# Turning the keys with packed matmuls in place of transposes, in a kernel of attention and two feed-forward layers

## The reference

```python
for t in range(S):
    cur = np.einsum('bhd,bhe->bhde', u[None] * kt, vt)
    y[:, :, t] = np.einsum('bhd,bhde->bhe', rt, state + cur)
    state = wt[:, :, :, None] * state + np.einsum('bhd,bhe->bhde', kt, vt)
```

## Time and profile before

| | |
|---|---|
| median of 3 runs | 1017.5 us (1017.02 to 1018.01) |
| profiled execution | 1017.5 us |
| its span | 1015.7 us |
| TensorE, matmuls | 994.5 us busy, 98% of the span |
| TensorE, weight loads | 971.7 us, 96% |
| vector engine | 559.8 us, 55% |
| scalar engine | 288.6 us, 28% |
| GpSimd | 24.4 us, 2% |
| mean granted TensorE clock | 0.998 |

### The profile page before, as it was taken

How to read it: one execution, slowest core, us unless ns; L and a number is a source line. 1 busy time by engine, 2 the same in 40 slices (tenths; PEclk the granted TensorE clock), 3 DMA queues, 4 the chain that set the end, 5 groups by cost and what they waited for, 6 DMA issues and landing times.

```text
span 1015.7 us, 27744 instructions
## 1 busy us (share of the span) xinstructions
PE 994.5 (98%) x11776; PEld 971.7 (96%) x11776; DVE 559.8 (55%) x1170; ACT 288.6 (28%) x604; POOL 24.4 (2%) x24
## 2 busy tenths in 40 slices
PE   5899999999999999999999999999999999999998
PEld 5799999999999999999999999999999999999998
DVE  7686655655656646556432437555545454555554
ACT  3435314223242241331222334222121222222212
POOL 4500000000000000000000000000000000000000
PEclk9999999999999999999999999999999999999999
DMA  6644401312113013110020413010101010101000
GB/s 162 167 135 120 117 14 35 109 30 64 53 29 92 25 31 91 52 38 2 26 60 1 138 35 125 1 47 1 47 1 47 1 46 0 46 4 43 15 11 24
DMA packets 42130, 52.96 MB, mean 52 GB/s; under 512 B 5152, under 2 KB 42016, under 8 KB 42016
## 3 DMA queue, kind: packets, MB, share of 16 engines
q1 hardware_dynamic: 40624, 51.04, 17.3%
q10 hardware_dynamic: 1392, 0.25, 0.2%
HBM read 39.48 MB, written 9.44 MB: 48 GB/s over the span
## 4 chain that ended last, share of the span: by engine, by line
PE 96%; DVE 1%; issue 1%; ACT 0%; ACTq 0%; DMA 0%; SPq 0%; DVEq 0%
PE products L166 18%; PE products L167 16%; PE products L168 16%; PE acc L168 12%; PE acc L166 12%; PE acc L167 12%; PE products L694 5%; PE products L736 1%; PE products L752 1%; PE products L671 1%; PE products L708 1%; PE products L721 1%; DMA x_parts<-f_y 0%; DVE k_in L927 0%; DVE a_sb L944 0%
## 5 line engine op out<-in xcount | busy, mean ns | idle before, releaser
L166 PE MATMUL products<-x_parts,weights_hi 128*128 128x384 f32 x576 | 200.9, 349 | 4.1 <-DMA x_parts<-f_y 1.9
L167 PE MATMUL products<-x_parts,weights_hi 128*128 128x384 f32 x576 | 194.2, 337 | 0.0
L168 PE MATMUL products<-x_parts,weights_lo 128*128 128x384 f32 x576 | 193.9, 337 | 0.0
L1235 DVE TENSOR_SCALAR leaky_low<-products,leaky_al 128x384 f32<-128x384 f32 x128 | 79.0, 617 | 169.4 <-PE products L168 169.3
L1095 DVE TENSOR_TENSOR g_sb<-a_g,products 128x384 f32<-128x384 f32 x96 | 53.2, 554 | 191.4 <-issue 129.5
L1182 ACT ACTIVATE leaky_g_hi<-leaky_g_sb 128x384 fp32r<-128x384 f32 x128 | 67.2, 525 | 295.0 <-DVE leaky_g_sb L1240 295.0
L514 ACT ACTIVATE g_hi<-g_sb 128x384 fp32r<-128x384 f32 x96 | 50.3, 524 | 254.1 <-DVE g_sb L1095 254.1
L166 PEld LDWEIGHTS products<-x_parts,weights_hi 128*128 128x128 f32 x576 | 108.1, 188 | 8.9 <-issue 5.3
L167 PEld LDWEIGHTS products<-x_parts,weights_hi 128*128 128x128 f32 x576 | 108.2, 188 | 0.0
L168 PEld LDWEIGHTS products<-x_parts,weights_lo 128*128 128x128 f32 x576 | 108.2, 188 | 0.0
L168 PE MATMUL acc<-g_hi,weights_lo 128*128 128x384 f32 x288 | 97.5, 338 | 0.0
(11 more groups left out here) (85 smaller groups left out, 1747.7 us busy)
## 6 DMA issues: line engine op xcount, KB each, us to landing
k_in<-in_k_dram SPq DMA_DIRECT2D x16, 336.0 KB, 3.9
r_in<-in_r_dram SPq DMA_DIRECT2D x16, 336.0 KB, 4.8
stage<-in_w_out_dram SPq DMA_DIRECT2D x14, 384.0 KB, 3.1
w_v<-in_v_dram SPq DMA_DIRECT2D x16, 288.0 KB, 3.5
y_dram<-x_in SPq DMA_DIRECT2D x8, 576.0 KB, 3.0
x_in<-y_dram SPq DMA_DIRECT2D x8, 576.0 KB, 4.4
out_dram<-leaky_out_sb SPq DMA_DIRECT2D x7, 576.0 KB, 3.3
stage<-in_w_dram SPq DMA_DIRECT2D x10, 336.0 KB, 3.8
```

The lines of the kernel that those rows point to most:

```text
L166: pe.matmul(out, w_hi, x_hi, start=first, stop=False)
L167: pe.matmul(out, w_hi, x_lo, start=False, stop=False)
L168: return pe.matmul(out, w_lo, x_hi, start=False, stop=last)
L1235: dve.tensor_scalar(self.low[f % 2][:, :], h, 0.0, self.al[:, f:f + 1], ALU.min, ALU.mult).then_inc(self.low_ready, 1)
```

## The change

The keys of a duo and stream were turned by six transposes, each of 112 channels x 128 positions against an identity of 112x112, giving 128 x 112 columns of PSUM, with three chunks in each of two banks. They are now turned by 24 ordinary matmuls: for each chunk, head and half, the 48x64 block of keys is the stationary operand, and a 48x48 identity on the same rows the moving one; the result is 64 positions x 48 columns. Each head has its own bank, with its chunks next to each other. The scalar engine's two copies of a stream therefore go by head and read 288 contiguous columns, where they had gone by half of the chunks and skipped the rows between the heads. The identity is loaded with two DMAs, one for the rows of each head, in place of one.

```diff
-        ident, leaf_mask = sb("ident", [ROWS, ROWS]), sb("leaf_mask", [P, BLOCK])
+        ident, leaf_mask = sb("ident", [P, D]), sb("leaf_mask", [P, BLOCK])
...
-                    for unit in range(2):
-                        copy(view(k_scratch[j], D * HALF * unit, [[D, HALF], [D * CH, 2], [1, D]], P),
-                             view(products, stream_bank(j, unit), [[ROWS, HALF], [64, 2], [1, D]], P)).then_inc(copied, 1)
+                    for hd in range(2):
+                        copy(view(k_scratch[j], D * CH * hd, [[1, D * CH]], P),
+                             view(products, stream_bank(j, hd), [[1, D * CH]], P)).then_inc(copied, 1)
...
-                act.dma_start(ident[:, :], constants[0:ROWS, 0:ROWS]).then_inc(ident_loaded, 16)
+                for hd in range(2):
+                    rows = slice(64 * hd, 64 * hd + 64)
+                    act.dma_start(ident[rows, :], constants[rows, 64 * hd:64 * hd + D]).then_inc(ident_loaded, 16)
...
-                        at = stream_bank(j, c // HALF) + ROWS * (c % HALF)
-                        last = pe.transpose(products[:, at:at + ROWS], k_in[j][:, c * P:(c + 1) * P], ident[:, :])
+                        for hd in range(2):
+                            for par in range(2):
+                                last = pe.matmul(view(products, stream_bank(j, hd) + D * c, [[1, D]], BLOCK, BLOCK * par),
+                                                 key_blocks(k_in[j], hd, c, par), ident[64 * hd:64 * hd + D, :], start=True, stop=True)
...
-                        pe.wait_ge(ident_loaded, 16)
+                        pe.wait_ge(ident_loaded, 32)
```

## The result

The changed kernel takes 1022.99 us (median of 5 runs, 1022.52 to 1023.82) against 1018.01 us for the kernel before in the same series. The ratio is 1.0052 with a 95% interval of 1.0041 to 1.0064: slower by 5.3 us, 4.2 to 6.5. Forecast were 4.3 us and 1021.8 us. The sign and the mechanism behind the start hold. The median of the five is 0.2 us inside the upper end of the range, 1023.2 us; the median of all 14 executions of the changed kernel in this series, 1023.37 us, lies 0.2 us above it.

A forecast was written before the change was run, and what follows sets the result against it. TensorE was taken as the bound, with 96% of the last-ending chain. Seven packets at 4.1 us, 0 for duo 0, copies and loads, and 0.25 us irregular waits made 4.3 us on 1017.5, so 1021.8 us; range 1019.8 to 1023.2 us.

The forecast's parts named there:

- the packet is paced by its weight columns: Turning packets of duos 1 to 7: 64 weight columns make each 2.10 us instead of 1.515, together 4.1 us more.
- Rival B: Turning packets behind the start: smaller moving operands give 1.93 us each, 2.9 us more in all, 1020.4 us; chance 0.08.
- E: Turning packets: quadrants overlap fully, each costs 1.57 us like the last level, 0.4 us more, 1017.9 us; chance 0.04.
- Copies, the second DMA for the identity, SBUF: Key copies hidden behind large matmuls, second identity load covered by 17 us, smaller tile without effect: 0 us.
- Irregular slots: Overlong packets between 50 and 512 us: a tenth more small instructions adds 0.25 us, bounds 0 and 1.9 us.
- Rival C: Gated stage: more waits on issue, two of the worst long packets met, 6.0 us more, 1023.5 us; chance 0.06.
- Duo 0: 0 us, with +0.4 as the upper bound: Turning packet in the start: costs the same as its transposes, 2.78 against 2.84 us; bounds -0.1 and +0.4 us.
- Rival D: Start's clock shifts: slow stretch at 34 to 38 us moves, half returns, 1.7 us, giving 1020.1 us; chance 0.06.
- The slow stretch of the earlier trace: TensorE from 34 to 38 us at mean granted clock 0.57; its disappearance would show the forecast wrong.
- The second half of D: Start: matmuls raise the clock where transposes do not, a further 1.2 us comes off, 1018.9 us; chance 0.02.

The follow-up runs named there:

- the two kernels with fewer columns: Changed kernel streaming only 16 of 48 moving columns, and changed kernel loading only 32 of 64 weight columns; single times 1026.82 and 1020.61 us.
- the partial kernels: Kernel before with packed matmuls only in duos 1 to 7 (ratio 1.0038), only in duo 0 (1.0025), or everywhere but stream 0 of duo 0 (1.0045).
- duo 0 alone: Kernel before with only duo 0's keys turned by packed matmuls; 1020.47 us, ratio 1.0025, and in a second series 1020.53 us, ratio 1.0021.
- transposes by head: Changed kernel with its packed matmuls replaced by one transpose per head and chunk, 24 a duo; 1016.93 us, ratio 0.9984, then 1017.45 us, ratio 0.9994.

## Why the prediction was right or wrong

- **TensorE is the bound behind the start, and the packet is paced by its weight columns.** Right, and shown: 2.09 to 2.10 us against the 2.10 taken, seven times; 7 x 0.58 = 4.1 us against a measured 3.9 for this part alone and 3.8 by the profiles. A small part of it is hidden, which I had not seen: in duo 1 the block behind the packet waits for the scalar engine's copy of a_g before, and not after, so that the step from turning to key_values grows by 6.47 - 6.16 = 0.31 us there, against 0.59 in duo 7 (6.47 against 5.88).
- **Rival B, paced as in the earlier trace rows, and E, paced as the last level.** Refuted by the same totals, and by the two kernels with fewer columns.
- **Copies, the second DMA for the identity, SBUF: 0.** The copies keep a mean of 413 ns in the profile after, as before. Packed duos 1 to 7 with the old load cost what the sum says within the interval, and nothing points at these terms.
- **Irregular slots, +0.25 us.** Not shown. In the profile after seven packets are longer than their kind, by 0.12 to 0.45 us, 1.6 us together; the two profiles of the kernel before have seven each, 2.5 and 2.2 us together. Their share did not grow with the instructions. Rival C, as I placed it, did not occur.
- **Duo 0: 0 us, with +0.4 as the upper bound.** This is the step that failed. It reads "The two kinds cost the same there, so I put this packet at 0". I compared durations on the array, 2.78 against 2.84 us, and they are right: without a standstill the packet took 3.02 us. What I left out is that it takes 192 instructions in place of 24, straight behind the levels' packets, where, as I read it, no block of large matmuls lets the supply catch up. A border between blocks of instructions, passed behind the turning in the kernel before, now lies inside it, and the next one inside key_values. Measured: 2.5 and 2.1 us (1.2 to 3.8). With the 3.9 us of the other duos that adds up to 6.0 to 6.4 us, more than the 5.3 of the whole change; the intervals of the parts are wide enough for this. I had the mechanism in hand, as rival C, and the earlier trace rows showed one such wait, but I spread it over the gated stage.
- **Rival D, the clock.** The clock of the start did shift, but no time came back. The slow stretch of the earlier trace rows is gone (the granted clock is shown as 1.00 from 34 to 38 us in the profile after), which the prediction had named as a sign of being wrong. 13 of the changed kernel's 14 executions have a mean granted clock of 1.000, against 6 of the 23 of the kernel before that ran beside the partial kernels.

  Yet the clock also rises later. The trace records the granted clock only from a certain moment on, and the views show 1.00 ahead of it. That moment is 30.99, 33.57 and 32.44 us in the three profiles whose duo 0 turns as before; it is 41.10 and 43.02 us in the changed kernel's two and 40.61 and 38.22 us in the two of duo 0 alone. The pace of TensorE changes with it: weighted_values needs 1.28 us to the first record behind its 48 in the profile after (36.23 to 37.51 us), and 0.68 us in the second profile of the kernel before (34.74 to 35.42). So up to there TensorE is at the lower of the two levels by its pace. The later rise alone is not the loss, since the transposes by head have it too (37.25 and 37.12 us) and are not slower than before.

  The second half of D, a start quickened by the new packet, did not occur. Slow stretches after the rise come in kernels with an unchanged duo 0 as well. In the kernel with packed duos 1 to 7 only, this window stands at 0.54:

```profile
43.00:50.00 7.00, 6.36 (x21) 0.54 0.92 233
```

  There large matmuls run 0.32 us apart in place of 0.17, which made that execution's start late although its duo 0 is that of before.

**What stays open** is how the 2.1 to 2.5 us of duo 0 divide. From the first record of the turning to the first of weighted_values it is 6.4 us in the kernel before, and 6.5 in its second profile and with duos 1 to 7 alone packed; with duo 0 packed it is 8.9 and 7.0 us in the two profiles of the changed kernel and 7.8 and 6.4 us in those of duo 0 alone. The mean of these four is 7.5, which makes 1.1 us. The slower pace until the later rise of the clock comes on top of it. A wait behind it takes some back: ahead of the first large matmul TensorE stands for 1.85, 2.11 and 3.42 us for the DMA of x_parts in the three profiles with duo 0 as before, and for at most 0.85 us in the four with duo 0 packed, which have a second such wait of 0.49 to 1.35 us. Single profiles cannot divide the 2.1 to 2.5 us among these. Open is also what decides when the fetch of a block starts. For the border inside the turning it started between 25.42 and 28.05 us in the profiles of the changed kernel, of duo 0 alone and of the two with fewer columns; in the earliest of these, the second one of duo 0 alone, the packet had landed at 27.08 us and the turning ran through.

## What to carry to other kernels

Price a packet of small matmuls by its weight columns first, against the nearest packet on the same quadrants, and take totals between the starts of its neighbours: that gave 2.10 us within 0.01. Then count its instructions, not only its time, where small matmuls follow small matmuls without large ones between: every 256 instructions TensorE needs a new block, and 192 instructions in place of 24 cost some 2 us at one such place, beside their time on the array nothing measurable at seven others. Whether a standstill on issue is of this kind can be read from when the instruction queue's packets land. And a second profile of the kernel before, taken ahead, would have shown how much of the start is chance.

## What the runs showed of the hardware that I had not expected

- In the kernels that pack both streams of duo 0, the standstills on issue of 0.35 to 2.32 us in the start come 256 TensorE instructions apart or a multiple of it, and each ends 1.2 to 1.5 us behind the landing of a packet of 16384 bytes on the instruction queue.
- In the start, matmuls of one kind run at two paces while the granted clock is shown as 1.00 for both: 96 records of key_values take 1.66 us in the earlier trace rows and 2.17 us in the kernel with transposes by head:

```profile
29.91 2.17 PE L724 MATMUL products<-w_v,k_scratch 64*48 64x48 f32 x96
```

  The first record of the granted clock stands at 30.99 us, inside the stretch of 1.66 us, and at 37.25 us in the other kernel. So the 1.00 shown ahead of it tells nothing on the pace; the durations do.
- Transposes of 48 rows on the two halves of the array overlap: two start 3 or 4 ns apart, and 24 of them take less than 12 with 112 rows. The Trainium skill, TensorEngine Tiling, section Restrictions, rules out a transpose of fp32 with column tiling; with row tiling alone it ran here.
